# One branch over both rare paths on TensorE, and six unread products instead of 21, in an attention, expert and feed-forward chain

## What is computed

```python
for t in range(S):                                   # attention, per batch and head
    S_re, S_im = ar * S_re - ai * S_im + k[t] v[t]^T, ar * S_im + ai * S_re
    y[t] = q[t] @ S_re

do_compute = x @ w_skip > 0                          # experts, x: 3072 x 384
e_idx = argmax(x @ w_gate); gate = softmax(x @ w_gate)[e_idx]
out = x;  out[rows of e] += gate * (relu(x[rows of e] @ w1[e]) @ w2[e])

h = x @ w_in;  out = (h * sigmoid(h)) @ w_out        # feed-forward, d_ff 2048
```

## Time and profile before

| | |
|---|---|
| median of 3 runs | 886.01 us (885.65 to 886.46) |
| profiled execution, its own time | 886.94 us |
| its span in the profile | 885.2 us |
| TensorE busy | 840.3 us (95%) |
| VectorE, ScalarE, GpSimd busy | 356.5, 347.6, 160.4 us |
| granted TensorE clock, mean | 0.991 of full |

### The profile page before, as it was taken

How to read it: one execution, slowest core, us unless ns; L and a number is a source line. 1 busy time by engine, 2 the same in 40 slices (tenths; PEclk the granted TensorE clock), 3 DMA queues, 4 the chain that set the end, 5 groups by cost and what they waited for, 6 DMA issues and landing times.

```text
span 885.2 us, 13266 instructions
## 1 busy us (share of the span) xinstructions
PE 840.3 (95%) x5224; PEld 749.8 (85%) x5224; DVE 356.5 (40%) x666; ACT 347.6 (39%) x606; POOL 160.4 (18%) x193
## 2 busy tenths in 40 slices
PE   1499999999999799999999999999999999999997
PEld 0278888898899579999998989989989998998997
DVE  1588878869774322333133122122122132122112
ACT  6888988888642121111112222222222222222221
POOL 2101121612403225466000001001001001001001
PEclk9899999999999999999999999999999999999999
DMA  9999879656423485999540000000000000000000
GB/s 170 159 192 238 116 98 125 116 87 82 118 110 127 139 178 186 206 250 273 162 136 1 1 0 36 1 1 36 1 1 36 1 1 36 1 1 29 8 1 36
DMA packets 174167, 77.34 MB, mean 87 GB/s; under 512 B 151592, under 2 KB 167304, under 8 KB 174096
## 3 DMA queue, kind: packets, MB, share of 16 engines
q1 hardware_dynamic: 169168, 60.54, 34.3%
q0 software_dynamic: 4928, 15.84, 6.3%
HBM read 60.80 MB, written 15.59 MB: 86 GB/s over the span
## 4 chain that ended last, share of the span: by engine, by line
PE 92%; DVE 2%; ACT 2%; issue 2%; DMA 1%; POOL 0%; SPq 0%; DVEq 0%; ACTq 0%; POOLq 0%
PE f_pU L1694 23%; PE f_pO L1700 22%; PE e_pH L1430 8%; PE e_pY L1444 8%; PE sc L513 5%; PE kvp L527 3%; PE tq L495 2%; PE tk L500 2%; PE yp L538 2%; PE yp L540 2%; PE cs L470 2%; PE cs L110 2%; PE cs L483 1%; PE cs L484 1%; PE e_pH L1479 1%
## 5 line engine op out<-in xcount | busy, mean ns | idle before, releaser
L1694 PE MATMUL f_pU<-f_xT,wi 128*128 128x512 f32 x864 | 215.1, 395 | 0.8 <-DVE f_xT L1635 0.8
L1700 PE MATMUL f_pO<-wo,gT 128*128 128x384 f32 x1152 | 213.8, 336 | 0.0
L1700 PEld LDWEIGHTS f_pO<-wo,gT 128*128 128x128 f32 x1152 | 202.6, 188 | 7.5
L1694 PEld LDWEIGHTS f_pU<-f_xT,wi 128*128 128x128 f32 x864 | 161.3, 188 | 32.5 <-DVE f_xT L1635 1.2
L1651 DVE TENSOR_TENSOR gT<-g,gT 128x512 fp32r<-128x512 f32 x96 | 66.5, 692 | 286.5 <-ACT gT L1678 279.4
L1673 ACT ACTIVATE g<-f_pU 128x512 f32<-128x512 f32 x96 | 57.5, 599 | 298.2 <-PE f_pU L1694 298.2
L1641 POOL DMA_INDIRECT out<-o,row_of x24 | 24.1, 1004 | 438.3 <-DVE o L1662 431.9
L1430 PE MATMUL e_pH<-e_xT,ring 128*128 128x224 f32 x384 | 74.0, 353 | 0.6 <-DVE e_xT L1543 0.6
L1444 PE MATMUL e_pY<-hT,ring 128*128 128x224 f32 x384 | 74.1, 353 | 0.0
L1430 PEld LDWEIGHTS e_pH<-e_xT,ring 128*128 128x128 f32 x384 | 72.6, 190 | 0.7 <-issue 0.7
L1444 PEld LDWEIGHTS e_pY<-hT,ring 128*128 128x128 f32 x384 | 72.1, 190 | 0.0
(11 more groups left out here) (194 smaller groups left out, 1023.1 us busy)
## 6 DMA issues: line engine op xcount, KB each, us to landing
ring<-in_moe_w SPq DMA_DIRECT2D x16, 1536.0 KB, 8.1
ring<-in_a_re SPq DMA_DIRECT2D x8, 576.0 KB, 8.4
ring<-in_a_im SPq DMA_DIRECT2D x8, 576.0 KB, 8.7
ring<-in_q SPq DMA_DIRECT2D x8, 576.0 KB, 8.2
ring<-in_k SPq DMA_DIRECT2D x8, 576.0 KB, 8.2
vraw<-in_v SPq DMA_DIRECT2D x8, 576.0 KB, 7.0
xs<-zero SPq DMA_DIRECT2D x9, 343.9 KB, 8.5
part<-in_moe_w_in POOLq DMA_DIRECT2D x12, 256.0 KB, 4.7
```

The costliest lines, as they stand in the source:

```text
L1694: mm = pe.matmul(pU[f % 2][:, :], wi[:, pw, c, f * 128:(f + 1) * 128], xT[b % 2][:, px, c, :], start=(k == 1), stop=(k == NK * len(TERMS)))
L1700: mm = pe.matmul(pO[t][:, 0:DM], gT[f % GB][:, pg, t * 128:(t + 1) * 128], wo[:, pw, f, :], start=(f == 0 and k == 0), stop=(f == NF - 1 a ...
```

## The change

VectorE writes one word more in `tabulate`: the sum of `mx` (how many further passes are asked for) and `weak`, a new word which is 1 if the flag's source is below 128. It is zero when neither rare part is wanted. TensorE waits for the table, loads this word, and branches once over everything rare: the flag's branch with the general path, and the passes. The experts' TensorE function is now issued twice, once with `odd` for the passes alone, and once without for the last pass. The other engines keep their two branches. Of the unread products, attention's last eight become five, and the 4 + 9 in the experts become one; the wait for `sent` between them goes.

```diff
-SETTLED_AT, COLS_AT, ROWS_AT, PASSES_AT, TAILS_AT = 0, 8, 136, 264, 268
+SETTLED_AT, COLS_AT, ROWS_AT, PASSES_AT, ODD_AT, TAILS_AT = 0, 8, 136, 264, 265, 268
...
+        self.weak = sb("weak", [1, 1])
...
         dve.tensor_scalar(table[0:1, PASSES_AT:PASSES_AT + 1], self.mx[0:1, 0:1], 1.0, None, ALU.add)
+        dve.tensor_tensor(table[0:1, ODD_AT:ODD_AT + 1], self.mx[0:1, 0:1], self.weak, ALU.add)
         link(dve.tensor_tensor(valid, valid, thr, ALU.mult))
...
             routing.count(pe, s, pC)
-            keep_busy(8)
+            keep_busy(5)
...
-                    dve.tensor_copy(flag, cs[1][0:1, 0:1]).then_inc(s["flag_done"], 1)
+                    dve.tensor_copy(flag, cs[1][0:1, 0:1])
+                    dve.tensor_scalar(routing.weak, cs[1][0:1, 0:1], 128.0, None, ALU.is_lt).then_inc(s["flag_done"], 1)
...
-        def tensor(pe):
+        def tensor(pe, odd):
...
-            passes(pe, body, lambda: pe.matmul(pX[0:1, 0, 0:1], ident[:, 0:1], ident[:, 0:1], start=True, stop=True))
-            keep_busy(4)
-            pe.wait_ge(after["sent"], 16 * routing.NT)
-            keep_busy(9)
-            body(0, last)
+            if odd:
+                passes(pe, body, lambda: pe.matmul(pX[0:1, 0, 0:1], ident[:, 0:1], ident[:, 0:1], start=True, stop=True))
+            else:
+                keep_busy(1)
+                body(0, last)
...
             att_run[2](pe)
-            pe.wait_ge(att["flag_done"], 1)
-            with pe.If(strong(pe)):
-                pe.wait_ge(gen["x_in"], 16)
-                agn_run[2](pe)
-                pe.wait_ge(agn["table_done"], 1)
-            exp_run[2](pe)
+            pe.wait_ge(att["table_done"], 1)
+            odd = pe.value_load(routing.table[0:1, ODD_AT:ODD_AT + 1], min_val=0, max_val=2 * PASSES)
+            with pe.If(odd > 0):
+                pe.wait_ge(att["flag_done"], 1)
+                with pe.If(strong(pe)):
+                    pe.wait_ge(gen["x_in"], 16)
+                    agn_run[2](pe)
+                    pe.wait_ge(agn["table_done"], 1)
+                exp_run[2](pe, True)
+            exp_run[2](pe, False)
             ffn_run[1](pe)
```

## The result

The changed kernel takes **882.38 us** (median of 6 runs, 882.14 to 883.17) against 886.07 (885.13 to 886.46, 6 runs); the ratio is 0.9961, 95% interval 0.9948 to 0.9974. It is faster by 3.7 us, not by the 6.9 forecast, and outside the range of 878.0 to 882.0. The profiled execution took 883.17 us, its span is 881.4.

A forecast was written before the change was run, and what follows sets the result against it. TensorE, working 95% of the span, was taken as the bound. The first up-projection 8.4 us earlier, less 1.5 for the clock, gave 6.9 off the median of 886.01: 879.1 us, range 878.0 to 882.0.

The forecast's parts named there:

- The first turn to the first up-projection: Handover to the experts: first turn at 306.05, first up-projection at 308.95 instead of 317.36, 8.4 us earlier.
- the cover that the jump was given: Handover: TensorE's jump and the product behind it end by 305.2 to 305.9, hidden by the rows' transfer until 306.01.
- What the clock takes back: First up-projection: half clock until 311.9 loses 1.5 us (0.4 to 2.5), leaving 6.9 of the 8.4 us.
- Rival A: Handover: clock returns late (dense stream only, 879.8 us) or early (turn counts, 878.7); chance 0.77 together with the forecast.
- What is late next: Idle turns after the first up-projection: their last rows land at 322.3, capping the gain at 7.3 us; nothing later binds.
- B: Handover: the jump takes 7 us and ends at 307.0; gain 4.7 us, 881.3; chance 0.10.
- C: Idle turns: their rows wait behind unit 3 and land at 327.0; gain 2.6 us, 883.4; chance 0.07.
- D: Experts: the clock stays at half until the first down-projection has ended; 12.0 us slower, 898; chance 0.02.
- E: Handover: the new word isn't zero and the branch doesn't jump; gain 2.5 us, 883.5; chance 0.01.
- F: Handover: something unseen holds the experts at 317; same time; chance 0.03.
- Nothing there turns up as a bound: After the idle turns: unit 3's load and GpSimd's splitting before feed-forward have slack, so a 7 us shift meets no bound.
- every shift of TensorE reaches the end of the kernel: From the first up-projection at 317.36 on, TensorE's shifts count in full if weights and rows come early enough.

The follow-up runs named there:

- the first experiment: The changed kernel with its new word in an unused column of the constants' tile, so that nothing moves in SBUF: 880.05 us, ratio 0.9926.

## Why the prediction was wrong

**The first turn to the first up-projection: right in its place, not in its terms.** Said 308.95, measured 308.32. The turn started at 305.95, as said (306.05), but behind the unread product and not behind the rows: these landed 0.6 us earlier than in the trace of before, and the cover that the jump was given was not there. What came out shorter is the way from the turn to the copy, 1.37 us (305.95 to 307.32) where 1.10 had been stretched to 1.95. The jump ended at 304.5, as said, though by other terms: the table's word took 0.73 us to load instead of 0.31, and the jump was 3.86 us, the lower of the two ends and not the upper one that I took.

**What the clock takes back: right in size, a little short.** The loss was put at 1.5 us with a clock back at 311.9; it came back at 312.6, and the up-projection took 11.52 - 9.32 = 2.2 us longer. The shorter turn (0.6) and the longer loss (0.7) cancel, and that 6.83 stands so near my 6.9 is in part luck. Rival A's later side (312.6 to 314.0, counted from the dense stream) is where it fell. But the first experiment, with the same program on TensorE, had its clock back at 309.7, on the early side and 1.7 us behind its first up product instead of 4.3: one trace doesn't decide whether the turn counts.

**What is late next: right at the handover.** The cap of 7.3 us was real: the fifth turn ran at 322.78, inside the 322.4 to 323.5 given, and in the first experiment, where TensorE came to it sooner, it waited for the transfer until 322.26. Rivals B, C, D, E and F didn't come.

**The failed step is the last sentence of that part, "Nothing there turns up as a bound", and with it the claim that every shift of TensorE reaches the end of the kernel.** The change was costed by its instructions: the added word as an operation of 0.14 us that VectorE hides. Its tile was not costed at all. It moves the weights by 32 bytes against the tiles that they are multiplied with, and 2016 records of feed-forward take 1.5 ns more on average, 3.0 us together. No row of feed-forward was read at all, though its pieces (2.08 to 2.10 us) stand in the trace of before; even those don't show what another placement costs, so a bound of zero on both sides was taken where a bound was missing. With the word elsewhere the forecast is off by 0.3 us, 6.9 against 6.6 measured, and this too is partly luck: in that run's trace the up-projection lost 0.8 us to the clock and not 1.5, and a wait of 1.2 us and a second stretch at half clock, which the prediction didn't have, took more than that back. The range failed with the sum: it took in late jumps, and no cost behind the experts.

## What to carry to other kernels

When a change adds a tile, even of four bytes, compare the addresses of the large tiles before and after, and compare the pace of the stages that the change doesn't touch. Put a small word into a tile that exists. And ask of unread products that keep TensorE awake whether they can run under a jump or a load of the sequencer, where they delay nothing, and what waits behind them: a gain is seen only up to the next transfer that lands.

## What the runs showed of the hardware

- The distance in SBUF between the two operands of a product changes its pace: 405.2 us for feed-forward at the old distance, 408.3 at 32 bytes less (up- and down-projections slower), 406.8 at 64 less (down-projections alone). It is the distance and not either address. Why, and what other distances would do, stays open; in the experts, whose left tiles moved too, the pieces of 9.08 and 9.10 us didn't change.
- The branch over the rare parts cost TensorE 3.3 to 4.6 us in all eleven traces, the corresponding ones on ScalarE and VectorE 45 to 72 ns. Products issued ahead of it run on: the array was busy to 303.95 while the sequencer jumped.
- At the handover the clock fell to half after each gap in the array of 3.90 us (the kernel before with the unused 1x1 tile) or more, and not after one of 3.16. In the first experiment it fell a second time, at 326.8, behind a wait of 1.2 us and four idle turns (rows below), and was low for 3.3 us. It fell there too in the changed kernel padded on both sides, behind a wait of 1.6 us, and not with 13 products ahead, behind one of 0.43; in the kernel before, the eight turns without a wait kept it.

```profile
322.30:326.70 4.40, 2.99 (x26) 1.00 0.82 183
326.80:330.10 3.30, 3.30 (x15) 0.50 1.06 380
```

- The slowest transfer of idle rows took 11.9 to 15.1 us to land in the ten traces with the 1792 row numbers issued behind it, and 11.6 in the one without. Whether the row numbers hold it up stays open.
